# Attention, gated convolution and spatial gating on one core: earlier first scores, paired rows of v, value groups cut in thirds, taps moved behind the last normalisation

## The reference

```python
k_sum = k.reshape(B, H, nb, block, D).max(axis=3)
v_sum = v.reshape(B, H, nb, block, D).mean(axis=3)
scores_l = scale * np.matmul(q, k.transpose(0, 1, 3, 2))
mask_l = np.abs(pos[:, None] - pos[None, :]) < window
scores_s = scale * np.einsum('bhsd,bhnd->bhsn', q, k_sum) + np.log(block)
a = softmax(concatenate([where(mask_l, scores_l, -1e9), scores_s]))   # with 1e-9 added to the sum
x = a @ concatenate([v, v_sum])
```

## Time and profile before

| | us |
|---|---|
| median of 3 runs | 313.92 (312.52 to 314.29) |
| the profiled execution | 311.59 |
| its span, first to last instruction | 309.5 |
| TensorE busy | 297.6 (96%) |
| VectorE busy | 171.5 (55%) |
| ScalarE busy | 153.8 (50%) |
| GpSimd busy | 116.1 (38%) |

### The profile page before, as it was taken

How to read it: one execution, slowest core, us unless ns; L and a number is a source line. 1 busy time by engine, 2 the same in 40 slices (tenths; PEclk the granted TensorE clock), 3 DMA queues, 4 the chain that set the end, 5 groups by cost and what they waited for, 6 DMA issues and landing times.

```text
span 309.5 us, 5418 instructions
## 1 busy us (share of the span) xinstructions
PE 297.6 (96%) x1820; PEld 275.0 (89%) x1820; DVE 171.5 (55%) x571; ACT 153.8 (50%) x471; POOL 116.1 (38%) x132
## 2 busy tenths in 40 slices
PE   7999999999869999899999999999999999999996
PEld 7898999999859999788899998888899999988885
DVE  5798898888668899972200005878755233320000
ACT  3789999999986664652212215343332212122221
POOL 6231575668532887360000000443477323320000
PEclk9999999999999999999999999999999999999999
DMA  8999998864710533000000001112110000012222
GB/s 172 237 213 224 232 203 184 214 176 107 196 51 0 154 120 102 2 0 1 0 2 0 2 0 51 51 53 68 35 36 0 0 2 0 0 36 79 90 104 102
DMA packets 51769, 25.53 MB, mean 82 GB/s; under 512 B 44554, under 2 KB 46878, under 8 KB 51742
## 3 DMA queue, kind: packets, MB, share of 16 engines
q1 hardware_dynamic: 51742, 25.18, 33.0%
HBM read 22.03 MB, written 3.15 MB: 81 GB/s over the span
## 4 chain that ended last, share of the span: by engine, by line
PE 73%; ACT 10%; DVE 8%; issue 5%; POOL 2%; DMA 1%; DVEq 0%; ACTq 0%; POOLq 0%
PE psum L662 57%; ACT probs L800 5%; DVE psum L1012 3%; PE psum L625 3%; PE psum L584 3%; PE psum L598 3%; PE psum L613 3%; PE psum L549 2%; PE psum L644 2%; ACT probsT L814 1%; ACT xT L822 1%; DVE work L1071 1%; PE psum L752 1%; DMA raw<-in_moe_w_in_dram 1%; DVE gate L1012 1%
## 5 line engine op out<-in xcount | busy, mean ns | idle before, releaser
L500 POOL TENSOR_TENSOR g_lo<-work,g_hi 128x384 fp32r<-128x384 f32 x32 | 32.3, 1026 | 35.9 <-ACT g_hi L926 26.3
L500 POOL TENSOR_TENSOR vn_lo<-work,vn_hi 128x512 fp32r<-128x512 f32 x12 | 15.5, 1293 | 72.9 <-DVE vn_hi L1108 72.9
L800 ACT ACTIVATE probs<-neg_s,neg_max 128x120 f32<-128x120 f32 x96 | 36.8, 387 | 1.4 <-DVE neg_max L945 1.2
L613 PE MATMUL psum<-probsT,v_win 120*128 120x128 f32 x192 | 29.5, 276 | 0.0
L584 PE MATMUL psum<-k_win,qT 128*128 128x120 f32 x192 | 29.0, 273 | 0.0
L945 DVE CUSTOM_DVE_ANT_0 neg_s<-psum,mask 128x120 f32<-128x120 f32 x96 | 24.6, 276 | 7.1 <-PE psum L584 7.1
L1012 DVE SCALAR_TENSOR_TENSOR psum<-xT,conv_c,psum 128x384 f32<-128x384 f32 x48 | 26.2, 615 | 2.8 <-ACT psum L841 2.8
L926 ACT ACTIVATE g_hi<-work 128x384 fp32r<-128x384 f32 x16 | 8.3, 523 | 34.8 <-DVE work L1120 34.8
L613 PEld LDWEIGHTS psum<-probsT,v_win 120*128 120x128 f32 x192 | 25.2, 191 | 0.3 <-ACT probsT L814 0.2
L584 PEld LDWEIGHTS psum<-k_win,qT 128*128 128x128 f32 x192 | 25.3, 191 | 0.0
L1086 DVE TENSOR_TENSOR wsp_lo<-psum,wsp_hi 128x384 fp32r<-128x384 f32 x12 | 6.6, 549 | 33.3 <-ACT wsp_hi L907 33.3
(11 more groups left out here) (123 smaller groups left out, 729.4 us busy)
## 6 DMA issues: line engine op xcount, KB each, us to landing
v_win<-in_v_dram SPq DMA_DIRECT2D x16, 240.0 KB, 3.0
k_nat<-in_k_dram SPq DMA_DIRECT2D x16, 192.0 KB, 4.5
q_nat<-in_q_dram SPq DMA_DIRECT2D x16, 192.0 KB, 3.7
v_nat<-in_v_dram SPq DMA_DIRECT2D x8, 384.0 KB, 4.7
out_dram<-work SPq DMA_DIRECT2D x11, 256.0 KB, 2.0
raw<-in_moe_w_spatial_dram SPq DMA_DIRECT2D x6, 384.0 KB, 3.2
raw<-in_moe_w_out_dram SPq DMA_DIRECT2D x8, 256.0 KB, 2.8
raw<-in_moe_w_in_dram SPq DMA_DIRECT2D x8, 256.0 KB, 3.0
```

The lines of the kernel that those rows point to most:

```text
L500: nc.gpsimd.tensor_tensor(dst_lo, src, dst_hi.bitcast(F32), ALU.subtract).then_inc(lo_sem, 1)
L613: ins = nc.tensor.matmul(bank_x(i)[:, i % 2 * 2 + g, :], v_win[0:KEYS, s, 2 * t + g, :], probsT[0:KEYS, i % 2, g, :], start=True, stop=True)
L800: ins = nc.scalar.activation(probs[:, i % RING, g, :], neg_s[:, i % 3, g, :], ACT.Exp, bias=neg_max[:, i % 4, g:g + 1], scale=-1.0, accum_ ...
```

## The change

- q of pair 0 is loaded in four transfers and not two: tiles 0 and 1 of both heads first (semaphore q_first), then the rest. TensorE turns the first piece only, issues scores(0), and turns the other two pieces behind them. The last 4 dummy transposes are dropped.
- GpSimd adds the rows of v in pairs, in place (add_v, one operation a pair of heads), and means(p) makes 3 products and not 6, waiting for v_nat_added. add_v(0) stands behind k_tails(0), add_v(p + 1) behind k_tails(p + 1).
- The second half of the middle x eviction of each pair goes from ScalarE to VectorE (take_x in steps i with i % 6 == 4).
- val(0) and val(1) are issued in the drain in thirds, one third in each of the steps 48 to 53, ahead of the turned probabilities.
- ScalarE's first tap of channel 0 goes from step 48 to 50, that of channel 1 from step 52 to its place in `between`. VectorE's taps in the drain are 2 in each of steps 51 to 53, where they were 12 over all eight steps.

```diff
-            sel = sb("sel", [P, RUN, KEYS], F32, early)
+            sel = sb("sel", [P, RUN // 2, KEYS], F32, early)
...
-            load_heads(0, q_h, q_nat, q_loaded, q_turned)
+            first = q_h[0:2].rearrange("h (t p) d -> p t h d", p=P)
+            for tiles, done in ((slice(0, 2), q_first), (slice(2, T), q_loaded[0])):
+                for h in range(2):
+                    sp.dma_start(q_nat[:, 0, tiles, h * D:(h + 1) * D], first[:, tiles, h]).then_inc(done, 16)
...
+            def add_v(p):
+
+                pool.wait_ge(v_nat_loaded[p % 2], 16 * (p // 2 + 1))
+                x = v_nat[:, p % 2, :, :].rearrange("p h (j e d) -> p h j e d", e=2, d=D)
+                nc.gpsimd.tensor_tensor(x[:, :, :, 0, :], x[:, :, :, 0, :], x[:, :, :, 1, :], ALU.add).then_inc(
+                    v_nat_added, 1)
...
             k_tails(0)
+            add_v(0)
             for p in range(PAIRS):
                 if p >= 2:
                     split_x(p - 2)
                 spread_means(p)
                 if p + 1 < PAIRS:
                     k_tails(p + 1)
+                    add_v(p + 1)
...
             def means(p):
 
-                pe.wait_ge(v_nat_loaded[p % 2], 16 * (p // 2 + 1))
+                pe.wait_ge(v_nat_added, p + 1)
...
-                for r in range(RUN):
-                    ins = nc.tensor.matmul(bank_m[0:KEYS], sel[:, r, :], v_nat[:, p % 2, :, r * D:(r + 1) * D],
-                                           start=(r == 0), stop=(r == RUN - 1))
+                for j in range(RUN // 2):
+                    ins = nc.tensor.matmul(bank_m[0:KEYS], sel[:, j, :], v_nat[:, p % 2, :, 2 * j * D:(2 * j + 1) * D],
+                                           start=(j == 0), stop=(j == RUN // 2 - 1))
...
-            for piece in range(PIECES):
-                turn_q(0, piece)
-            keep_warm(WARM[2])
+            turn_q(0, 0)
...
                 if i == 0:
+                    for piece in range(1, PIECES):
+                        turn_q(0, piece)
...
-                if STEPS + 3 <= i < STEPS + 3 + VALS_IN:
-                    val(i - STEPS - 3)
+                if i >= STEPS:
+                    n, term = divmod(i - STEPS, 3)
+                    val(n, (term,))
...
-                nc.scalar.activation(by_group(x_of(p, r * P, 2 * P)[D:P]), bank_x(2 * j)[D:P, :, GROUP:P],
-                                     ACT.Copy).then_inc(xB_ready, 1)
+                if j % 3 != 1:
+                    nc.scalar.activation(by_group(x_of(p, r * P, 2 * P)[D:P]), bank_x(2 * j)[D:P, :, GROUP:P],
+                                         ACT.Copy).then_inc(xB_ready, 1)
...
+            def take_x(j):
+
+                dve.wait_ge(x_summed, 2 * j + 2)
+                p, r = divmod(2 * j, T)
+                nc.vector.tensor_copy(by_group(x_of(p, r * P, 2 * P)[D:P]),
+                                      bank_x(2 * j)[D:P, :, GROUP:P]).then_inc(xD_ready, 1)
...
+                if i >= 8 and i % 6 == 4:
+                    take_x((i - 8) // 2)
...
-DRAIN_TAPS = (1, 1, 2, 2, 1, 1, 2, 2)
-FIRST_AT = (48, 52)
+DRAIN_TAPS = (0, 0, 0, 2, 2, 2, 0, 0)
+FIRST_AT = (50,)
 V_DMAS = 6
-WARM = (15, 8, 4)
+WARM = (15, 8)
```

More of the change, by code:

```diff
@@ L240, in wait_x @@
         def wait_x(eng, tiles):
-            eng.wait_ge(xA_ready, tiles // 2)
-            eng.wait_ge(xB_ready, tiles // 2)
+            n = tiles // 2
+            eng.wait_ge(xA_ready, n)
+            eng.wait_ge(xB_ready, n - (n + 1) // 3)
+            if n >= 2:
+                eng.wait_ge(xD_ready, (n + 1) // 3)
         def rows(w, n, cols=slice(None)):
@@ L545, in turn @@
                 n = len(loaded)
-                if piece == 0:
+                if p == 0 and src is q_nat:
+                    pe.wait_ge(loaded[0] if piece else q_first, 2 * 16)
+                elif piece == 0:
                     pe.wait_ge(loaded[p % n], 2 * 16 * (p // n + 1))
@@ L650, in _, with product @@
             keep_warm(WARM[1])
-            for piece in range(PIECES):
-                turn_q(0, piece)
-            keep_warm(WARM[2])
-            def product(o, lhs, rhs, low=None):
+            turn_q(0, 0)
+            def product(o, lhs, rhs, low=None, terms=range(3)):
                 n = len(lhs[0])
-                for part, (a, b) in enumerate(((0, 0), (1, 0), (0, 1))):
+                for part in terms:
+                    a, b = ((0, 0), (1, 0), (0, 1))[part]
                     if part == 2 and low:
@@ L663, in product @@
                                                stop=(part == 2 and c == n - 1))
-                ins.then_inc(group_done, 1)
+                if part == 2:
+                    ins.then_inc(group_done, 1)
             def by_k(w, cols=slice(None)):
@@ L672, in g_tiles, with val @@
                                                             [low(b * C + k) for k in range(C)])]
-            def val(n):
+            def val(n, terms=range(3)):
                 c, w = channels(n)
                 b, c = divmod(c, C)
-                if n % (2 * C) == 0:
-                    pe.wait_ge(x_split, (b + 1) * C)
-                    pe.wait_ge(w_split, n_split(W_OUT - 1))
-                wait_bank("val", n)
+                if 0 in terms:
+                    if n % (2 * C) == 0:
+                        pe.wait_ge(x_split, (b + 1) * C)
+                        pe.wait_ge(w_split, n_split(W_OUT - 1))
+                    wait_bank("val", n)
                 m = slice(c * P, (c + 1) * P)
                 product(bank("val", n, HALF), [by_k(wval_hi, m), by_k(wval_lo, m)],
-                        [[x_hi[:, b * C + k, w] for k in range(C)], [x_low(b * C + k)[:, w] for k in range(C)]])
+                        [[x_hi[:, b * C + k, w] for k in range(C)], [x_low(b * C + k)[:, w] for k in range(C)]],
+                        terms=terms)
             def fused(n):
@@ L1123 @@
 RING = 6
-VALS_IN = 1
+VALS_IN = 2
 WVALS_OF = ((), (), (), (0,), (1,), (2,), (3,), ())
```

9 lines of the change are left out of this document (6 added, 3 removed).

## The result

The changed kernel takes 319.66 us (median of 4 runs, 319.09 to 320.31), the kernel before 314.11 us in the same comparison (4 runs, 312.52 to 314.85): 1.018 of it, 95% interval 1.014 to 1.023. It is slower by 5.5 us, where the prediction said 5.5. The profiled execution took 319.96 us with a span of 318.2 us.

A forecast was written before the change was run, and what follows sets the result against it. It took the attention pairs as bound by nearly full TensorE, ScalarE and VectorE, the end by VectorE's taps and gates. Terms +0.95 + 5.95 - 1.06 - 0.3 = +5.5 us on the 313.92 median gave 319.4 us, range 316.0 to 322.8.

The forecast's parts named there:

- Means 3 to 7: Attention pairs: TensorE's means wait for GpSimd's add, +1.19 us a pair over five steps, +5.9 us.
- The loop: Attention pair: means, ScalarE's evictions, GpSimd's split, spread, tails and add, next means; 11.14 us against 9.95.
- Rival 1: Attention pairs: the wait on the add is covered and ScalarE sets the pair; about 310.1 us, chance 0.07.
- The start: Kernel start up to means 2: early gain lost, means 1 later, half coming back; +0.95 us (0 to +2).
- rival 5: Attention pairs: TensorE's clock falls in the new stops; 326 us or more, chance 0.03.
- Means 7 to the drain: ScalarE's stretch from means 7 to the first taps: shorter means and one x half dropped, -1.06 us.
- a sign of being wrong: At fused group 0: the prediction is wrong if it moves by another amount than means 7 less 1.4 us.
- Drain and taps: Drain: TensorE's thirds don't count; VectorE's taps start 2.6 us later but meet fewer stalls; -0.3 us (-2 to +2.6).
- The x half: Eviction moved from ScalarE to VectorE: 0.40 us off ScalarE, worth nothing while the add's wait binds, paying only in the last pair.
- Rival 2: Drain: the later taps are not made good, all stalls stay; about +3 us, 322.3 us, chance 0.15.
- The 1.49 us stall: VectorE's wait in the drain for GpSimd's release of a work buffer; claimed to go, since VectorE gets there later.
- The base: Whole kernel: +5.5 us gives 317.1 on the profiled 311.59 us; laid on the median 313.92, 2.3 higher, it gives 319.4.

The follow-up runs named there:

- add alone: The kernel before with only the paired add on GpSimd, placed behind the k tails as in the change: 321.79 us, 1.025 of before.
- nearly free add: The changed kernel with the add over one column of each head, order and waits unchanged, sums incomplete: 313.89 us, one run.
- the kernel with the add ahead: The changed kernel with the add moved in GpSimd's queue, ahead of the x split (pairs 1 and 2: ahead of the k tails): 308.20 us, 0.983 of before.
- the filled stop: The changed kernel with eight idle-filling transposes on TensorE ahead of means 1: 318.59 us.
- drain and taps alone: The kernel before with only the drain's thirds of val groups and the later taps: 310.89 us, 0.994 of before.
- the start alone: The kernel before with only the new start (q transfers, scores 0 behind the first turned piece, no last warm group): 312.26 us, 1.000 of before.
- the add ahead and the first tap earlier: The changed kernel with the add moved ahead of GpSimd's x split, and ScalarE's first tap at step 48 instead of 50: 308.54 us.
- two adds ahead: The changed kernel with the add moved ahead of GpSimd's x split and a second same-size instruction behind each add: 309.87 us, one run.

## Why the prediction was right, and where it was not

**Means 3 to 7, the term that decided.** Right. The loop was put at 11.14 us and measured at 11.21; five steps at +1.26 are +6.3 against +5.95. The add took 0.99 us where 1.03 was taken from the subtract in the earlier trace rows; GpSimd's part from its start to the add's was 5.33 (5.31 predicted). The misses are small: x to the split 0.12, add to means 0.10, means to the eviction behind them 1.14 against 1.07. The stops of TensorE are 1.67 us, said to be some 2. The add alone and the nearly free add show the loop as cause, and moving the add shows the place as cause. The Trainium skill's figure (GPSIMD Engine Reference, Performance versus the Vector engine: 4497 ns for 2048 elements), from which the estimate of 0.84 us came, was 0.15 us too low here. The prediction has the trace agree with the ratio of about two that the Trainium skill gives; its own rows make it 1.03 to 0.64, which is 1.6. The Trainium skill's advice for two inputs, VectorE, wasn't tried; what helped was a place in GpSimd's idle time.

**Rival 1**, the covered add, was given 0.07 because GpSimd's idle time lies ahead of the chain. That is right for this order of the queue, and it is also the remedy: put the add into that idle time, and rival 1's gain comes out: it was put at 3.8 us, and the kernel with the add ahead is 3.8 under before, by the profiled executions (307.82 and 311.59) and by the medians of its comparison (308.20 and 312.03). Its 310.1 was laid on a base 1.9 us higher.

**The start.** Mis-sized: +0.95 for means 2, +2.43 in the trace. Means 0 were put at some 12.5 and came at 11.45; means 1 were put at 17.2 and came at 16.59 (+1.4, not +2.0). That half of their delay comes back was wrong. Three things took its place. The clock fell behind the stop at means 1, where rival 5 looked only at the later pairs; means 2 stand 27.48 - 26.43 = 1.05 us behind those of the kernel with the filled stop. Then pair 2's k was turned 0.7 us later than in before (18.59, 17.85), after a wait of 0.42 for its landing, and the prediction had not looked at that transfer at all, though in before too TensorE waits for it. And the add holds means 2 as well: it stands behind the last k tail, ends at 27.38, and means 2 start at 27.48; from the turn of k to means 2 it is 26.43 - 18.27 = 8.16 us with the filled stop, 7.1 to 7.3 in the kernels without that loop. In the execution with the filled stop means 2 are +1.38. Before and the drain and taps alone, which have the same start, differ by 0.73 at means 2, so parts of this size are read from one execution each and are no more exact than that.

**Rival 5.** The clock did fall, once in the execution and not in every pair. The Trainium skill (TensorE: Matmul & The Clock Gate, HAM oscillation) tells of a loop whose wait in each turn is longer than its work. Here TensorE works 9.33 us of 11.22, and the later pairs ran at 1.00, so the prediction, where it says that by that rule the rival wins, took the rule further than the Trainium skill does.

**Means 7 to the drain.** Right in size for the mechanism, and missing a term: 1.06 us were to be gained on ScalarE, with 0.3 behind it, -1.36 in all. The profile of the changed kernel has +0.04, those of the filled stop and of the nearly free add, which change nothing there, 53.60 and 53.59 us, so -1.07 and -1.08. In the changed kernel's execution SyncE's issue of a transfer of v took 1.87 us at 87.04, ahead of the two issues of w_out; with the filled stop the same line took 0.56 at that place, as in before. So the piece of w_out came late and TensorE waited 1.69 us for it, where it was 0.42 in before. It was the same with the add alone (1.64). So the loop doesn't bring this wait by itself, since it is there with the filled stop too. How many of the changed kernel's other runs have it isn't known, and why the issue takes long there wasn't tried. The prediction had named as a sign of being wrong that fused group 0 moves by another amount than means 7 less 1.4. In the changed kernel's profile means 7 move by 8.72 and fused group 0 by 8.76, so that sign came; with the filled stop it is 7.59 and 6.52.

**Drain and taps.** Right in size by the profile alone, and incomplete. -0.3 was predicted, -0.12 measured with drain and taps alone. What the medians gain at equal clock, 0.9, stays open. Rival 2, the tail that pays in full, didn't come. Behind the add's loop the new drain looks worth more, 56.74 - 54.71 = 2.0 us between the add alone and the changed kernel. There the old taps stand twice, 2.74 us for ScalarE's copy and 1.64 for GpSimd's release, 1.25 and 1.49 in the earlier trace rows; with the late taps it is 2.91 ahead of the first tap, 0.38 and 0.16. But the loop isn't needed for the 2.74: the start alone, which has no add, stands 2.75 us at the same place and takes 55.95, and what the two share is a fall of the clock in the old drain (0.56 and 0.59 from 100 to 104 us with the add alone). That the fall makes the stall is read from these two profiles; no run filled that stop. The x half of the last pair, worth 0.4 by the prediction, is in the 2.0 as well. The 1.49 us stall goes, as predicted.

**The x half.** Right: under the loop it buys nothing. It buys nothing at the old pitch either, where TensorE's own row binds; with the add ahead its worth is open.

**The base.** The sum came out at +5.5 us on the trace and was laid on the median, 2.3 us over the profiled execution. On the trace the change is +8.4 to +8.7, so the sum missed some 3 us of it; on the medians it is +5.5. Some 2 of these 3 us are the fall of the clock at means 1 and the late w_out piece: the profile with the filled stop has neither, and has +1.38 up to means 2, +6.21 in the five pairs and -1.07 behind them, +6.5 at fused group 0 against +5.5 predicted.

Before's runs, too, differ among themselves, with the mean granted clock. Of 35 of its runs, taken beside my experiments, 19 are at 1.000 (311.05 to 312.31 us, median 311.5), 6 at 0.994 or 0.995 (312.42 to 314.64) and 10 at 0.988 or 0.989 (313.41 to 314.82); its profiled execution is one at 1.000. The clocks of the four runs of before in the result's comparison aren't on record, but all four (312.52 or more) lie above every run at 1.000. So its median of 313.92 held, by this, some 2 us of lower clock that its trace does not show. The changed kernel has 0.994 or 0.995 in each of its four runs, and by the two groups of the filled stop its 319.66 holds some 1.6; the add alone has 0.989 in each of four. Both at full clock it is 317.8 (the two such runs with the filled stop) against 311.4 (the six such runs of before beside them), +6.4 us. That the number came out within 0.3 us is in part luck, since two errors met: the sum was too low by the start and the w_out piece, and the base it was laid on was high by the clock.

## What the runs showed of the hardware that I had not expected

**The clock falls at two places of this kernel, in some runs.** One fall goes with 1.6 us in the changed kernel (the two groups of runs with the filled stop) and in before (medians of 311.5 at 1.000 and 313.1 at 0.994 or 0.995); with the add ahead and the first tap earlier it doesn't show (308.29 to 309.76 with it in three runs, 308.32 without in one). One place is behind the stop at means 1. The other is in the drain. The page's row of granted clocks in 40 slices, of the changed kernel, the add alone and the start alone in this order, shows where:

```profile
PEclk9979999999999999999999999999999999999999
```

```profile
PEclk9979999999997999999999999999999999999999
```

```profile
PEclk9999999999988999999999999999999999999999
```

The third slice is the start, the 12th and 13th are the drain. In the profile of the kernel with the new start alone (old drain), TensorE waited 1.43 and 1.42 us, was busy 0.58 of 2 us between 90 and 92, and then:

```profile
90.00:92.00 2.00, 0.58 (x7) 0.42 (x5) 1.06 (x4) 1.65 (x4) 1.47 (x2) 0.95 0.01 4
92.00:94.00 2.00, 2.00 (x9) 2.00 (x10) 2.00 (x6) 1.02 (x3) 1.16 (x1) 0.50 0.00 0
94.00:96.00 2.00, 2.00 (x10) 2.00 (x9) 2.00 (x5) 0.00 (x0) 0.00 (x0) 0.69 0.00 0
```

The same stops of 1.43 and 1.42 us stand in before, with the same 0.58 of 2 us busy between 90 and 92, and there the clock stayed at 1.00. So the trace shows that it can fall behind them, not that it must.

With the thirds in the drain and no add, 15 of 16 runs have a mean clock of 0.999 or more, where of the kernel before 19 of 35 do, and of the start alone, with the old drain, 7 of 10. This fits a use of thirds that the prediction didn't see: "it doesn't count, since VectorE is what fused group 0 waits for" left out what a busy TensorE does for its clock. What it takes away are the longer runs, not the 0.9 us by which drain and taps alone are faster at equal clock. It is an inference from the spread of runs. The thirds with the old taps were run only with the add ahead (three of four runs at 1.000, one at 0.993), not on the kernel before, and where a fall stands in an unprofiled run isn't on record.

**The length of a stop didn't decide alone.** Ahead of means 1 the clock fell behind stops of 2.62 (add alone), 2.17, 1.83 and 1.70 us (add ahead, first tap earlier) and not behind 1.69, 1.71 and 1.74; in the pairs it never fell behind 1.67.

**Issues of the same line can differ threefold and more.** In the changed kernel the issue of v's rows took 0.56 us in one pair of heads and 1.87 in another; with two adds ahead one of that line took 4.07. At the same place of nearly the same kernel it was 1.87 and 0.56 (changed, and changed with the filled stop). Who waits is whatever stands behind it in SyncE's queue.

## What to carry to other kernels

An operation that lightens the busiest engine and goes to a lightly loaded one is priced by where it stands in that engine's queue: follow the queue from its last wait to the operation and on to who needs it, and close the loop; if it is longer than the pitch, look for the engine's idle time and put the operation ahead of that wait (here 319.7 us became 308.2 with the same work). An operation that is moved up meets the next limit, here the landing of its own input and the k tails behind it. Ahead of a start-up edit, look for the transfer that all later work waits for. And set the mean clock of each run beside its time before one profiled execution is taken as the base of a sum, and look at a second execution before a wait that only one shows is given a cause.
